# First chunk by pairs with a score bank each, and the loop's scores one tile later

## What is computed

```python
scores = scale * np.matmul(q_c, k_c.transpose(0, 1, 2, 4, 3))     # blocks of 64 positions
scores = scores - np.max(scores, axis=-1, keepdims=True)
attn = np.exp(scores)
attn = attn / (np.sum(attn, axis=-1, keepdims=True) + 1e-09)
out = np.matmul(attn, v_c)
...
xn = (x - mu) / np.sqrt(var + 1e-06) * g_ln
ch = np.maximum(xn @ w_ch1, 0.0) @ w_ch2
x = x + ch
...
h = np.maximum(x @ w_in, 0.0)
gate = 1.0 / (1.0 + np.exp(-conv_out))      # conv_out: h, three taps along the positions
return (h * gate @ w_out)
```

## Time and profile before

| | before |
|---|---|
| median of 3 runs | 1373.87 us (1373.07 to 1373.87) |
| the profiled execution | 1372.77 us, of it span 1370.9 us |
| PE busy in the span | 1321.6 us (96%) |
| DVE, ACT, POOL busy | 698.8, 380.3, 177.4 us |
| first 60 us: PE busy, mean granted clock | 29.54 us, 0.74 |
| a chunk of the loop (265.42 to 365.30) | 99.88 us, PE busy 99.42 |

### The profile page before, as it was taken

The page is one execution under the profiler, slowest core; times in us unless marked ns, Lnnn a source line. Parts: engine busy times, 40 slices in busy tenths (PEclk is TensorE's granted clock), DMA queues, the critical chain, the costliest instruction groups (busy, mean ns, idle before and its releaser), DMA issues.

```text
span 1370.9 us, 20558 instructions
## 1 busy us (share of the span) xinstructions
PE 1321.6 (96%) x8376; PEld 1121.4 (82%) x8376; DVE 698.8 (51%) x944; ACT 380.3 (28%) x606; POOL 177.4 (13%) x137
## 2 busy tenths in 40 slices
PE   4699999999999999999999999999889999999999
PEld 4478888888888888888888888888779899999997
DVE  4643533534543533634534535213976686676671
ACT  2442322312312312312212313112532333233330
POOL 1442000000000000000000000310632232222230
PEclk8699999999999999999999999999999999999999
DMA  9111011020020110110110100303101101201101
GB/s 338 47 47 47 31 46 46 31 69 23 31 69 23 46 53 23 54 46 23 54 54 14 54 23 0 127 0 126 37 8 59 49 32 57 73 15 50 39 16 54
DMA packets 30636, 69.62 MB, mean 51 GB/s; under 512 B 2448, under 2 KB 2448, under 8 KB 30608
## 3 DMA queue, kind: packets, MB, share of 16 engines
q1 hardware_dynamic: 25856, 59.79, 12.4%
q10 hardware_dynamic: 4752, 9.44, 1.8%
HBM read 50.35 MB, written 18.87 MB: 50 GB/s over the span
## 4 chain that ended last, share of the span: by engine, by line
PE 91%; DVE 7%; DMA 1%; ACT 1%; issue 1%; SPq 0%; DVEq 0%
PE ps L375 28%; PE ps L377 27%; PE ps L376 27%; PE ps L421 3%; PE ps L394 3%; DVE conv L847 2%; PE ps L406 1%; DVE prob L726 1%; DVE row_sum L720 1%; DVE y_second L836 1%; DVE conv L844 0%; DMA k_sb<-in_kk 0%; DVE hl L773 0%; DVE xc L762 0%; DMA x_scratch<-x_cur 0%
## 5 line engine op out<-in xcount | busy, mean ns | idle before, releaser
L773 DVE SCALAR_TENSOR_TENSOR hl<-ps,hh 128x512 fp32r<-128x512 f32 x144 | 99.5, 691 | 359.0 <-ACT hh L580 359.0
L375 PE MATMUL ps<-xnh,w1h 128*128 128x512 f32 x576 | 229.2, 398 | 4.4 <-DVE xnl L768 4.4
L375 PE MATMUL ps<-hh,w2h 128*128 128x512 f32 x576 | 227.4, 395 | 0.0
L377 PE MATMUL ps<-xnh,w1l 128*128 128x512 f32 x576 | 225.3, 391 | 0.0
L376 PE MATMUL ps<-xnl,w1h 128*128 128x512 f32 x576 | 225.2, 391 | 0.0
L377 PE MATMUL ps<-hh,w2l 128*128 128x512 f32 x576 | 224.5, 390 | 0.0
L376 PE MATMUL ps<-hl,w2h 128*128 128x512 f32 x576 | 224.1, 389 | 0.0
L580 ACT ACTIVATE hh<-ps 128x512 fp32r<-128x512 f32 x144 | 86.0, 597 | 452.4 <-PE ps L377 452.4
L847 DVE SCALAR_TENSOR_TENSOR conv<-h_pad,cw_sb,conv 128x576 f32<-128x576 f32 x128 | 144.1, 1125 | 1.4
L358 POOL TENSOR_TENSOR conv<-h_pad,conv 128x576 f32<-128x576 f32 x64 | 105.3, 1645 | 263.2 <-ACT conv L661 263.2
L375 PEld LDWEIGHTS ps<-xnh,w1h 128*128 128x128 f32 x576 | 108.5, 188 | 28.8 <-DVE xnl L768 4.6
(11 more groups left out here) (97 smaller groups left out, 1945.9 us busy)
## 6 DMA issues: line engine op xcount, KB each, us to landing
qv_sb<-in_qv SPq DMA_DIRECT2D x34, 512.0 KB, 3.3
x_scratch<-x_cur ACTq DMA_DIRECT2D x9, 1024.0 KB, 4.3
y_raw<-x_scratch SPq DMA_DIRECT2D x8, 1152.0 KB, 5.7
out<-o_sb SPq DMA_DIRECT2D x36, 256.0 KB, 2.0
k_sb<-in_kk SPq DMA_DIRECT2D x34, 256.0 KB, 3.5
w_raw<-in_w SPq DMA_DIRECT2D x8, 1024.0 KB, 13.6
wi_raw<-in_w_in SPq DMA_DIRECT2D x1, 2048.0 KB, 7.5
wo_raw<-in_w_out SPq DMA_DIRECT2D x1, 2048.0 KB, 8.4
```

The source lines that it names most:

```text
L375: nc.tensor.matmul(o, wh, xh, start=first, stop=False)
L377: return nc.tensor.matmul(o, wl, xh, start=False, stop=last)
L773: nc.vector.scalar_tensor_tensor(hl[:, f % RING, :], ps_hid(f), 0.0, hh[:, f % RING, :].bitcast(F32), ALU.max, ALU.subtract).then_inc(hl_d ...
```

## The change

**Prologue.** Each of the four pairs has a score bank of its own (SCO, HID, HID + 1, ACC + 3), so `scores` no longer waits for a subtraction. Odd pairs are turned into another bank (ACC + 2). The layer norm runs by pairs on 128 columns (`pair_cols`). `first_mean` and `first_var` take the four feature groups straight from `x_next` and `square` in four accumulating fp32 matmuls of 128 columns, in the used-up score bank of the pair, in place of sums on DVE. The copy of values to `x_next` goes from DVE to ACT. All these steps, each a function per pair, stand in an order written out for each engine. 30 matmuls on the identity instead of 18 stand before the loop, with a wait for the last `xnl` behind them. 6 weight casts stand before the loop; `some_his(2)` per tile of chunk 0 stays. All four pairs are loaded ahead of the first weights.

**Loop.** SCORE_AT moves from 2g + 1 to 2g + 2, and the turns and values with it: scores at 2, 4, 6, 8, turns at 3, 5, 7, 9, values at 4, 6, 8, 10. The sum over feature groups is made on DVE behind each pair's copy (`reduce_sum`, as line 818 did in the prologue), and `sum_tiles(.., x_next, 1)` with its three adds at tile 10 is gone. The adds of the squares remain.

```diff
-WARM = 18
-
-SCORE_AT = {2 * g + 1: g for g in range(GP)}
+WARM = 30
+
+SCORE_AT = {2 * g + 2: g for g in range(GP)}
...
+    def ps_turn(c, gl_):
+        n = ACC + 2 if isinstance(c, int) and c == 0 and gl_ % 2 else ATT
+        return ps[:, n, :]
...
-        n = HID if isinstance(c, int) and c == 0 and gl_ % 2 else SCO
+        n = (SCO, HID, HID + 1, ACC + 3)[gl_] if isinstance(c, int) and c == 0 else SCO
...
                 load_group(0, gl_)
-                if gl_ == 1:
-                    load_w1(0)
-                    load_w2(0)
+            load_w1(0)
+            load_w2(0)
...
-                need(pe, sub_done, gl_ - 1 if isinstance(c, int) else c * GP + gl_)
+                if not isinstance(c, int):
+                    pe.wait_ge(sub_done, c * GP + gl_)
...
+            def first_mean(n):
+
+                pe.wait_ge(x_done, n + 1)
+                for k in range(KC):
+                    mm = nc.tensor.matmul(ps_first_mean(n), ones[:, :].bitcast(F32), x_next[:, k, pair_cols(n)],
+                                          start=k == 0, stop=k == KC - 1)
+                mm.then_inc(mean0_done, 1)
...
             for _ in range(WARM):
-                nc.tensor.matmul(ps[:, HID + 1, 0:P], ident[:, :], ident[:, :], start=True, stop=True)
+                nc.tensor.matmul(ps[:, ATT, 0:P], ident[:, :], ident[:, :], start=True, stop=True)
+            pe.wait_ge(xnl_done, GP)
...
+            def first_x(n):
+                act.wait_ge(value_done, n + 1)
+                nc.scalar.copy(x_next[:, :, pair_cols(n)],
+                               ps_val(0, n).rearrange("p (k n) -> p k n", k=KC)).then_inc(x_done, 1)
...
+            first_x(1)
+            first_square(0)
+            take_turned(0, 2)
+            first_x(2)
+            first_square(1)
+            first_std(0)
+            take_turned(0, 3)
+            some_his(1)
+            first_x(3)
+            some_his(1)
+            first_std(1)
+            first_square(2)
+            first_hi(0)
+            first_std(2)
+            some_his(1)
+            first_hi(1)
+            first_square(3)
+            first_std(3)
+            some_his(2)
+            first_hi(2)
+            some_his(1)
+            first_hi(3)
...
-            def sum_tiles(c, src, n):
-
-                base = (n - 1) * (KC - 1)
+                dve.wait_ge(x_done, c * GP + gl_ + 1)
+                nc.vector.reduce_sum(ln_sum[:, cols], x_next[:, :, cols].rearrange("p k n -> p n k"),
+                                     AX_X).then_inc(group_summed, 1)
...
+            less_max(0, 0)
+            less_max(0, 1)
+            normalise(0, 0)
+            less_max(0, 2)
+            normalise(0, 1)
+            less_max(0, 3)
+            normalise(0, 2)
+            first_centre(0)
+            normalise(0, 3)
             dve.wait_ge(small_in, 32)
-            scale_by_rstd(0)
-            split_xn(0)
+            first_centre(1)
+            first_scale(0)
+            first_centre(2)
+            first_scale(1)
+            first_lo(0)
+            first_centre(3)
+            first_scale(2)
+            first_lo(1)
+            first_scale(3)
+            first_lo(2)
+            first_lo(3)
```

More of the change, by code:

```diff
@@ L173, in build, with pair_cols, ps_first_mean, ps_first_var @@
     ps_mean = ps[:, SCO, 0:NT]
-    ps_att = ps[:, ATT, :]
+    def pair_cols(n):
+        return slice(n * G2, (n + 1) * G2)
+    def ps_first_mean(n):
+        return ps_score(0, n)[:, 0:G2]
+    def ps_first_var(n):
+        return ps_score(0, n)[:, G2:2 * G2]
     def ps_gate(f):
@@ L430, in feature_mean, with first_var @@
                 nc.tensor.matmul(ps_mean, ones[:, :], ln_lo[:, :], start=False, stop=True).then_inc(done, 1)
-            def first_mean(done):
-                nc.tensor.matmul(ps_mean, ones[:, :].bitcast(F32), ln_sum[:, :], start=True, stop=True).then_inc(done, 1)
+            def first_mean(n):
[4 more added lines that the diff above has]
+                mm.then_inc(mean0_done, 1)
+            def first_var(n):
+                pe.wait_ge(sq0_done, n + 1)
+                for k in range(KC):
+                    mm = nc.tensor.matmul(ps_first_var(n), ones[:, :].bitcast(F32), square[:, k, pair_cols(n)],
+                                          start=k == 0, stop=k == KC - 1)
+                mm.then_inc(var0_done, 1)
             def up(j, f):
@@ L483, in _ @@
             scores(0, 1)
[L484 to L494, removed]
+            turn(0, 0)
+            scores(0, 2)
+            values(0, 0)
+            turn(0, 1)
+            scores(0, 3)
+            first_mean(0)
+            values(0, 1)
+            turn(0, 2)
+            first_mean(1)
+            first_var(0)
+            values(0, 2)
+            turn(0, 3)
+            first_var(1)
+            first_mean(2)
+            values(0, 3)
+            first_var(2)
+            first_mean(3)
+            first_var(3)
             for _ in range(WARM):
-                nc.tensor.matmul(ps[:, HID + 1, 0:P], ident[:, :], ident[:, :], start=True, stop=True)
+                nc.tensor.matmul(ps[:, ATT, 0:P], ident[:, :], ident[:, :], start=True, stop=True)
+            pe.wait_ge(xnl_done, GP)
             with pe.Fori(0, NC - 1) as j:
@@ L801, in chunk @@
                         if f == SQSUM_AT:
-                            sum_tiles(j + 1, square, 2)
+                            sum_squares(j + 1)
                         if f == VAR_AT + 1:
@@ new lines, in first_scale @@
+            def first_scale(n):
+                cols = pair_cols(n)
+                dve.wait_ge(std0_done, n + 1)
+                nc.vector.reciprocal(rstd[:, cols], rstd[:, cols]).then_inc(rstd0_done, 1)
+                dve.wait_ge(rstd0_done, n + 1)
+                for k in range(KC):
+                    mul = nc.vector.scalar_tensor_tensor(xc[:, k, cols], xc[:, k, cols], g_sb[:, k:k + 1], rstd[:, cols],
+                                                         ALU.mult, ALU.mult)
+                mul.then_inc(xn0_done, 1)
```

105 lines of the change are left out of this document (53 added, 52 removed).

## The result

| | before | changed |
|---|---|---|
| median | 1373.87 us (1373.07 to 1374.12) | 1351.65 us (1350.98 to 1352.68) |
| ratio | | 0.984, 95% interval 0.9823 to 0.9857 |
| profiled execution, span | 1370.9 us | 1349.4 us |
| first up-projection matmul | 59.87 us, half clock | 47.60 us, full clock |
| last down-projection matmul | 948.6 us | 928.1 us |

A forecast was written before the change was run, and what follows sets the result against it. PE, busy 96% of the span, was taken as the bound, with gains only where it stands still or runs at half clock. 1373.87 - 13.1 (prologue) - 6.5 (loop) = 1354.3 us; range 1349.5 to 1361.

The forecast's parts named there:

- the two places named: Prologue before PE's first up-projection at 59.87 us, and one PE stall at tile 2 in each of eight attending chunks.
- The loop, 6.5 us: Loop, turn at tile 2: scores one tile later remove stalls, 7 x 0.66 + 1.84 in chunk 0 = 6.5 us.
- Rivals 3 and 5: Loop: wait only moves, 1360.8 us, chance 0.09; extra sum makes turns wait in each chunk, slower, 1398 us, chance 0.03.
- The prologue's walk: Prologue, step by step through the queues: up-projection starts at 47.1 us, 48.6 with a clock relapse; gain 13.1 us.
- the 0.8 us to spare: End of prologue: last pair's scaling, cast and lo end at 46.3 us, warm-up matmuls on PE at 47.1.
- Rivals 4 and 6: Prologue: ScalarE becomes bound, 1360.3 us, chance 0.10; pairs don't overlap, loop's gain eaten, within 0.2%, chance 0.02.
- rival 2: Prologue: PE's clock stays low until the warm-up matmuls, start 56.5, gain 5.2 us; time 1362.2 us, chance 0.10.
- The relapse ahead of variance 2: Prologue: PE's clock falls again in idle gaps before variance 2 or 3, costing 0.8 to 2.2 us, 1.5 taken.
- rival 1: Prologue: PE's clock never falls once it has risen, start 47.1, 1.5 us earlier; time 1352.8 us, chance 0.24.
- The prediction's last sign: Prologue: the mechanism is wrong if PE's clock is half between 30 and 45 us.
- Priced at nothing: Prologue: first weights' DMAs issued behind all groups were taken to cost or gain nothing, with pairs 2 and 3 landing earlier.
- the free edits: Prologue and chunk 0: 6 weight casts before the loop rather than 13, and first weights' DMAs later, each priced at nothing.

## Why the prediction was right, and where it was off

- **The bound.** Right for 20.5 of the 21.5 us: they came from the two places named, and PE had no wait in the loop behind them.
- **The loop, 6.5 us.** Right in size and kind: 1.8 in chunk 0, 4.7 in the seven others. Nothing else became late: exp came 0.77 us later (0.8 forecast), normalising not at all. Rivals 3 and 5 fall with that; the shift alone gave 5.9 us without the sums.
- **The prologue's walk.** Turn 2 at 25.62 (25.6), end of values 33.98 (33.6), end of variance 3 40.64 (40.3), up-projection 47.60 (47.1). Pair 1's transfer, 8.51 instead of 8.2, had been made up by turn 2, since turn 1 ran at full clock; the 0.4 came behind it. The length of the identity matmuls, 6.86 us, was 6.9 by the record rate. Mis-sized was what runs beside them: the last pair's scaling took 3.56 us where 2.3 were taken, so the last `xnl` was ready at 47.24 and not 46.3, and of the 0.8 us to spare 0.1 was left. Had it been longer still, the start would have been late; that it was not is luck. Rivals 4 and 6 fall.
- **The clock.** It was full from 24.4 on, so rival 2 falls. The relapse ahead of variance 2, 1.5 us taken, did not happen in this execution. Three other executions with the same code up to there had it, at the gap named, for 1.4 to 1.7 us: its size was right, that it comes every time was not. By the number the nearest is therefore rival 1 (1352.8, measured 1351.65), but its mechanism, a clock that never falls once it has risen, is not what happened: the clock fell at 21.0 behind turn 1. There it cost the walk nothing, which had it at half clock up to about 24 anyway. The prediction's last sign, wrong if the clock is half between 30 and 45, contradicts its own relapse, which lies in that stretch. Rival 1's rule of the Trainium skill ("TensorE: Matmul & The Clock Gate", section "Why this matters for your kernels"), that only gaps above about 3 us matter, does not hold in the rows: gaps of 1.93, 1.99 and 2.91 us were followed by half clock.
- **What was missing.** The second half. Its 422.3 us were taken as fixed, and it gave 1.0. The other runs put it at 421.1 to 424.6 with the same code, by the time at which one store lands and by spells of half clock behind PE's gaps; that is as large as several terms of my sum.
- **Priced at nothing.** The order of the first transfers. The walk assumed pair 2 landed in time, which is only so because of that edit: without it, scores 2 wait 0.67 us, and that is its price as far as shown. It belonged to the gain, not to the free edits.

Of 19.6 forecast and 21.5 measured in the span: prologue with clock 13.1 against 12.3 + 1.7 = 14.0, loop 6.5 against 6.5, second half 0 against 1.0. The 0.9 between 13.1 and 14.0 are the relapse that was taken and not met, 1.5, less a start 0.5 later than the walk's and 0.1 of clock.

## What to carry to other kernels

A stall that only the first step of a pipeline has can often be removed by starting one step later, if a whole stage then stands in between; read the slack from the steps that are already covered. In a chain through in-order queues, walk every queue: where one engine's queue holds the next unit's first step in front of this unit's last, one late link is passed on to both. Compare experiments at a landmark ahead of any stage that varies by itself; here the total hid differences of 1.7 us that the first half showed plainly. Take more than one profile before a term of 1 or 2 us is believed: the same code gave first halves of 928.1 and 930.3.

## What the runs showed of the hardware

The same kernel, at the same gap of 1.99 us of PE, lost the clock in one execution and kept it in the other; over ten executions with this gap three lost it, and it cost 1.4 to 1.7 us of the start of the loop. Filling a gap of 4.75 us with 4.2 us of matmuls whose results nobody uses kept the clock full; the second half took 419.9 us with it, 421.3 and 421.5 in the changed kernel's two executions. The relu that waits for one store of the same size started 4.33 us behind its issue in most executions of the changed kernel and up to 6.22 in others. Four scalings of 128 columns on DVE took 1.14 us with POOL idle and 3.56 us with POOL at weights.
